# Joining the two parts of x on VectorE before the residual's transposing passes

## The chip, the cores and the metric

The kernel runs on one core of a Trainium2 chip. The metric is the device time of one execution in microseconds. Each number below is from the runs of this kernel or from one profiled execution of it.

## What is computed

Three blocks follow each other: a recurrence over 768 positions (8 heads of 48), a mixing block and a gated convolution block. Only the second one's first half matters here. x is the output of the recurrence, 768 positions by 384 features, for each of 4 batches:

```python
xt = x.transpose(0, 2, 1)
h = np.maximum(xt @ w_tok1, 0.0) @ w_tok2
u = x + h.transpose(0, 2, 1)
h2 = np.maximum(u @ w_ch1, 0.0) @ w_ch2
return u + h2
```

All of it is float32. The kernel gets float32 accuracy out of the faster fp32r products by splitting a tensor into a high part (the value rounded to fp32r) and a low part (what was rounded off): a product is high by high, high by low and low by high, three passes in the place of one.

## The kernel before, in words

TensorE (PE) does all products, ScalarE (ACT) writes high parts, VectorE (DVE) writes low parts, GpSimd (POOL) does the recurrence's states, SyncE (SP) issues loads. Each engine walks the same hand-written list of words, `PROGRAM`: a prologue, a `TRIP` that runs for b = 1, 2, 3, and a `TAIL`. A trip holds the recurrence of batch b beside the dense blocks of batch b - 1, so four batches of dense work lie in trips 1, 2, 3 and the tail. The order on each engine is fixed by that list; semaphores hold an engine at an instruction until another has done its part.

Words that matter here:

- `Z:s` writes x of one super unit (256 positions) to `xs`, high part by ACT and low part by DVE (L614). `xs` is [128, 2, 6, 384]: positions on the partitions, part, position block, feature.
- `G1.0.g` (g = 0, 1): the first product of batch b (`token_products`, L816). ACT and DVE then write the parts of `h1` (on DVE it is L619, tile h).
- `U.j.0` (j = 0, 1, 2, a tile of 256 positions): u transposed, features on the partitions, in three feature blocks `dt`. PE does for each `dt` 6 products of `h1` and the weight `tok2` (tiles tok,h) and then adds the residual: 4 transposing matmuls by the identity (tiles ident,xs), one for each of two position blocks and each of the two parts of x (L847 to L851). Feature blocks 0 and 1 share a PSUM bank, 2 has the next one; `mm_done` is raised after blocks 1 and 2. ACT then writes the high part of `us` (n = 0 for blocks 0 and 1, n = 1 for block 2) and DVE its low part (L632).
- `C1.j.g`, `C2.j.g` (g = 0..5): the two products with `ch1` and `ch2`, with the low part of `hid` by DVE (L619) between them. `C1.j.0` uses the PSUM bank that `U.j`'s n = 0 used, so PE can't begin it before DVE has written `us` low for n = 0 (`ring_free`).
- `X.j.0`: u + h2 into `xf` (DVE L647, L651, L653) and its parts `x2s` (ACT, DVE L657). `tap`, `gate`, `V`, `M`, `S`, `O`: the third block; DVE L670 does the taps, `V` is a product on PE, `M` multiplies it with the gate on DVE (L539, gate) and has ACT write a high part, `S` is DVE's low part, `O` the last product on PE (tiles outw,x2s), which needs both.
- `L1` to `L32`, `T`: levels of the recurrence. PE does 64 small products (tiles rk); DVE then scales r and k (L539, tiles rk or rk_next, called the scaling step below) and writes `at` (L594). PE's next level of the same super unit waits for the scaling step.

Around the change the list reads: in a trip `... G1.0.0 tap.2.1 tap.2.2 G1.0.1 V.2.0 tap.2.3 gate.2.0 M.2.0 tap.2.4 ... L4:3 O.2.0`, then at the start of the next one `L8:0 U.0.0 L16:0 C1.0.0 L32:0`; in its middle `X.0.0 L8:1 U.1.0 L16:1 C1.1.0 tap.0.0 L32:1`; later `X.1.0 U.2.0 T:2 tap.1.0 C1.2.0`. In the tail there are no levels: `U.0.0 C1.0.0`, `X.0.0 U.1.0 tap.0.0 tap.0.1 C1.1.0`, `X.1.0 U.2.0 tap.1.0 tap.1.1 C1.2.0`. The first `G1` (batch 0) stands at the end of the prologue.

Of the kernel before, what the change touches and what calls it, by code (L numbers as in the profile page):

```python
# [12 lines left out]
DM = H * D  # L13
# [174 lines left out]
def build(nc, rk, v, w, u, mask_d, ident_d, tok1_d, tok2_d, ch1_d, ch2_d, val_d, conv_d, outw_d, y_out):  # L188
    ctx = ExitStack()
    with ctx:  # L190
        def sb(name, shape, dt=F32):
            return ctx.enter_context(nc.sbuf_tensor(name, shape, dt))

        def sem(name):
            return ctx.enter_context(nc.semaphore(name))
# [35 lines left out]
        with ExitStack() as early:  # L231
            homes += [home_of_a_super_unit(early, 1), home_of_a_super_unit(early, 2)]
        xs = sb("xs", [P, 2, UNITS, DM], F32R)
        h1 = sb("h1", [P, 2, FT // P, DM], F32R)
# [38 lines left out]
        y_half, y_done = sem("y_half"), sem("y_done")  # L273
        xh_done, xl_done = sem("xh_done"), sem("xl_done")
        mm_done = sem("mm_done")
        ring_free = [sem("ring_free0"), sem("ring_free1")]
# [23 lines left out]
        def ring_filled(use):  # L300

            return use + 1
# [234 lines left out]
        def _(dve):  # L537
# [59 lines left out]
            def att(s, name):  # L597
# [12 lines left out]
                elif name == "Z":  # L610
# [5 lines left out]
                        .then_inc(xl_done, 1)  # L616

            def relu_low(out, bank, hi):
                return nc.vector.scalar_tensor_tensor(out, bank, 0.0, hi.bitcast(F32), ALU.max, ALU.subtract)  # L619

            def dense(b, kind, j, g):
                if kind == "G1":
                    use = RING_USE[(b, "G1", 0, g)]
                    need(dve, h1_hi, since(b, 2, g + 1))
                    relu_low(h1[:, LO, g, :], ps[:, RING + use % 2, 0:DM], h1[:, HI, g, :])\
                        .then_inc(ring_free[use % 2], 1)
                elif kind == "U":
                    for n, dts in ((0, slice(0, 2)), (1, slice(2, 3))):
                        use = RING_USE[(b, "U", j, n)]
                        need(dve, u_hi, since(b, 2 * TILES, 2 * j + n + 1))  # L630
                        bank = ps[:, RING + use % 2, 0:(2 - n) * TT].rearrange("p (d t) -> p d t", t=TT)
                        nc.vector.tensor_tensor(us[:, LO, dts, :], bank, us[:, HI, dts, :].bitcast(F32),  # L632
                                                ALU.subtract).then_inc(ring_free[use % 2], 1)
                elif kind == "C1":
                    use = RING_USE[(b, "C1", j, g)]
# [59 lines left out]
        def _(pe):  # L695
# [131 lines left out]
            def dense(b, kind, j, g):  # L827
# [7 lines left out]
                elif kind == "U":  # L835
                    ready = RING_USE[(b, "G1", 0, 1)]
                    need(pe, ring_free[ready % 2], ring_read(ready))
                    for dt in range(DT):
                        if dt == 2:
                            use = RING_USE[(b, "U", j, 1)]  # L840
                            need(pe, ring_free[use % 2], ring_read(use - 2))
                        bank = ps[:, RING + use % 2, dt % 2 * TT:(dt % 2 + 1) * TT]
                        rows = (lambda a, kt: h1[:, a, kt, dt * P:(dt + 1) * P],
                                lambda a, kt: wcols("tok2", a, kt * S + j * TT, TT))
                        hi_terms(bank, range(FT // P), *rows, True, True)
                        lo_terms(bank, range(FT // P), *rows, True, False)
                        for sc in range(2):  # L847
                            for part in (HI, LO):
                                ins = mm(bank[:, sc * P:(sc + 1) * P],
                                         xs[:, part, 2 * j + sc, dt * P:(dt + 1) * P].bitcast(F32), ident[:, :],  # L850
                                         False, is_transpose=True)  # L851
                        if dt:
                            ins.then_inc(mm_done, 1)
                elif kind == "C1":
# [136 lines left out]
```

## Time and profile before

| | |
|---|---|
| median of 3 runs | 670.53 us (670.13 to 674.12) |
| the profiled execution's own time | 670.57 us |
| its span, first to last instruction | 668.8 us |
| PE busy | 618.1 us (92%) |
| DVE busy | 390.7 us (58%) |
| ACT busy | 177.7 us (27%) |
| POOL busy | 97.0 us (15%) |
| mean granted TensorE clock | 0.990 |
| transposing matmuls on x | 144, from 99.3 to 618.2 us |

PEld is TensorE's weight load, which overlaps PE. Matmuls are pipelined, so the time that one takes from PE is the distance between the starts of neighbours and not its duration. A timeline row merges neighbours of one kind (x4 is four of them).

### The profile page before, as it was taken

What the parts mean: (1) busy time and instruction counts of PE and PEld (TensorE: products, weight loads), DVE (VectorE), ACT (ScalarE), POOL (GpSimd) and SP (SyncE); (2) the same over time, 40 slices, a digit from 0 to 9 for tenths busy, and PEclk for the clock granted to TensorE, in tenths of its full rate; (3) what the DMA queues carried; (4) which work ended last, traced back from release to release, by engine and by line L of the source; (5) the groups of instructions that cost most, each with busy time, mean ns of one, the idle gap of its engine ahead of it and who ended that gap; (6) DMA issues with size and microseconds to landing.
All of it is one profiled execution on the core that took longest, in us unless ns stands there. A gap on an engine that the chain in (4) does not pass through costs nothing.

```text
span 668.8 us, 24044 instructions
## 1 busy us (share of the span) xinstructions
PE 618.1 (92%) x11188; PEld 593.7 (89%) x11188; DVE 390.7 (58%) x609; ACT 177.7 (27%) x306; POOL 97.0 (15%) x110
## 2 busy tenths in 40 slices
PE   3588689999998999999998999999999999999995
PEld 2587679989998999999998999999999999999995
DVE  4894495495767284485768285385767152443524
ACT  2113324223232132122232132213222131222313
POOL 2214633303002000303003000403002000000000
PEclk9999989999999999999999999999999999999997
DMA  9811552400301200310400300210000000000000
GB/s 238 253 51 51 165 158 84 120 5 11 123 4 50 82 2 26 83 28 3 116 18 24 109 1 27 58 52 3 2 26 2 25 25 1 1 2 25 2 25 24
DMA packets 13331, 35.27 MB, mean 53 GB/s; under 512 B 1584, under 2 KB 7984, under 8 KB 11888
## 3 DMA queue, kind: packets, MB, share of 16 engines
q1 hardware_dynamic: 9776, 29.01, 15.6%
q10 hardware_dynamic: 3456, 4.72, 2.0%
q8 instruction: 88, 1.44, 0.9%
q14 instruction: 11, 0.09, 0.0%
HBM read 29.01 MB, written 4.72 MB: 50 GB/s over the span
## 4 chain that ended last, share of the span: by engine, by line
PE 79%; DVE 11%; issue 4%; ACT 2%; DMA 2%; POOL 1%; SPq 0%; DVEq 0%; ACTq 0%; POOLq 0%
PE ps L697 79%; DVE gate L670 3%; DVE at L594 2%; DMA w<-in_w_dram 2%; DVE rk L539 2%; DVE hid L619 1%; DVE wp L539 1%; DVE rk_next L539 1%; ACT x2s L429 1%; DVE us L632 1%; POOL st L412 1%; POOL st L415 1%; DVE xf L647 0%; DVE xf L651 0%; ACT hid L488 0%
## 5 line engine op out<-in xcount | busy, mean ns | idle before, releaser
L697 PE MATMUL ps<-us,ch 128*128 128x256 f32 x1296 | 167.1, 283 | 1.4 <-DVE us L632 0.8
L697 PE MATMUL ps<-hid,ch 128*128 128x256 f32 x1296 | 167.1, 283 | 0.0
L697 PEld LDWEIGHTS ps<-us,ch 128*128 128x128 f32 x1296 | 157.1, 188 | 4.8 <-DVE us L632 2.0
L697 PEld LDWEIGHTS ps<-hid,ch 128*128 128x128 f32 x1296 | 157.3, 188 | 1.9 <-issue 0.2
L619 DVE SCALAR_TENSOR_TENSOR hid<-ps,hid 128x512 fp32r<-128x512 f32 x72 | 49.8, 691 | 134.9 <-ACT hid L488 134.9
L488 ACT ACTIVATE hid<-ps 128x512 fp32r<-128x512 f32 x72 | 42.9, 597 | 153.5 <-PE ps L697 153.5
L594 DVE COPY_PREDICATED at<-masks,ps 128x512 f32<-128x512 uint8 (+1 forms) x72 | 65.3, 911 | 23.1 <-PE ps L697 23.1
L670 DVE SCALAR_TENSOR_TENSOR gate<-xf,cw,gate 128x256 f32<-128x256 f32 x144 | 73.1, 555 | 2.9 <-ACT gate L504 2.0
L697 PE MATMUL ps<-rk 48*64 48x32 f32 (+1 forms) x2240 | 48.8, 243 | 12.4 <-issue 8.8
L697 PEld LDWEIGHTS ps<-rk 48*64 48x64 f32 (+1 forms) x2240 | 44.9, 162 | 17.0 <-issue 14.7
L412 POOL TENSOR_TENSOR st<-st,wp 112x192 f32<-112x192 f32 x40 | 25.5, 638 | 207.5 <-ACT ds L429 200.8
L539 DVE TENSOR_TENSOR rk<-rk,wp 112x1024 f32<-112x1024 f32 x35 | 44.1, 1260 | 12.1 <-PE ps L697 12.1
L697 PE MATMUL ps<-x2s,val 128*128 128x256 f32 x324 | 41.6, 284 | 6.5 <-DVE hid L619 4.9
L697 PE MATMUL ps<-outw,x2s 128*128 128x384 f32 x216 | 43.1, 355 | 4.4 <-ACT x2s L429 4.4
L697 PEld LDWEIGHTS ps<-x2s,val 128*128 128x128 f32 x324 | 39.9, 191 | 7.4 <-DVE hid L619 5.6
L697 PEld LDWEIGHTS ps<-outw,x2s 128*128 128x128 f32 x216 | 39.6, 200 | 5.0 <-DVE gate L539 4.7
L539 DVE TENSOR_TENSOR rk_next<-rk_next,wp 112x1024 f32<-112x1024 f32 x25 | 30.9, 1235 | 12.1 <-PE ps L697 12.1
L697 PE MATMUL ps<-tok,h 128*128 128x256 f32 x216 | 34.3, 294 | 0.6 <-DVE h L619 0.5
L429 ACT ACTIVATE x2s<-xf 128x512 fp32r<-128x512 f32 (+1 forms) x24 | 11.3, 516 | 69.5 <-DVE xf L651 69.5
L697 PE MATMUL ps<-fk 48*64 48x64 f32 x768 | 18.2, 252 | 11.9 <-DMA ident<-in_ident_dram 9.9
L697 PEld LDWEIGHTS ps<-tok,h 128*128 128x128 f32 x216 | 28.0, 189 | 1.2 <-issue 0.6
L697 PEld LDWEIGHTS ps<-rk_next 48*64 48x64 f32 (+1 forms) x1600 | 23.8, 129 | 5.9 <-issue 3.8
(72 smaller groups left out, 614.1 us busy)
## 6 DMA issues: line engine op xcount, KB each, us to landing
rk<-in_rk_dram SPq DMA_DIRECT2D x7, 896.0 KB, 6.6
vs<-in_v_dram SPq DMA_DIRECT2D x12, 384.0 KB, 7.4
out_dram<-gate ACTq DMA_DIRECT2D x24, 192.0 KB, 3.6
rk_next<-in_rk_dram SPq DMA_DIRECT2D x5, 896.0 KB, 6.1
w<-in_w_dram SPq DMA_DIRECT2D x7, 448.0 KB, 7.9
gate<-in_moe_w_ch_dram SPq DMA_DIRECT2D x6, 384.0 KB, 3.3
xf<-in_moe_w_ch_dram SPq DMA_DIRECT2D x6, 384.0 KB, 3.2
w_next<-in_w_dram SPq DMA_DIRECT2D x5, 448.0 KB, 7.7
```

Source lines behind the costliest of these rows:

```text
L412: nc.gpsimd.tensor_tensor(new, now, decay[:, :, q].unsqueeze(2).to_broadcast([RD, PAIRS, D]), ALU.mult).then_inc(st_decayed, 1)
L415: nc.gpsimd.tensor_tensor(new, new, ds[0:RD, q], ALU.add).then_inc(st_done, 1)
L429: return nc.scalar.activation(out, in_, ACT.Copy)
L488: nc.scalar.activation(hid[:, HI, g % 2, :], ps[:, RING + use % 2, :], ACT.Relu)\
L539: return nc.vector.tensor_tensor(out, a, b_, ALU.mult)
L594: nc.vector.copy_predicated(out, may.unsqueeze(1).to_broadcast(list(out.shape)), src)\
L619: return nc.vector.scalar_tensor_tensor(out, bank, 0.0, hi.bitcast(F32), ALU.max, ALU.subtract)
L632: nc.vector.tensor_tensor(us[:, LO, dts, :], bank, us[:, HI, dts, :].bitcast(F32), ALU.subtract).then_inc(ring_free[use % 2], 1)
L670: nc.vector.scalar_tensor_tensor(gate3[:, dt, :], xf[:, dt, k:k + TT], cw[:, dt, k:k + 1], gate3[:, dt, :], ALU.mult, ALU.add).then_inc(ta ...
L697: return nc.tensor.matmul(out, lhsT, rhs, start=start, stop=stop, skip_group_check=True, **kw)
```

## The change

`x_sum` is a float32 tensor of [128, 6, 384] that gets the same place in SBUF as the high part of `xs`. A new function `join_x(b, j)` writes one third of it (2 position blocks, 128x768 elements) on DVE as high part plus low part; it waits for the last product of `G1`, which reads the high part. Piece 0 is done right behind `G1.0.1`'s low part, pieces 1 and 2 right behind the low parts of `U.0.0` and `U.1.0`: 12 additions in all. In `U` the products of both feature blocks of a bank come first and the transposing matmuls behind them, one per position block on `x_sum` in the place of two on `xs`: 72 in the place of 144. PE waits for the piece (`x_joined`) before the transposing matmuls.

```diff
+        with ExitStack() as joined:
+            x_sum = joined.enter_context(nc.sbuf_tensor("x_sum", [P, UNITS, DM], F32))
         xs = sb("xs", [P, 2, UNITS, DM], F32R)
...
+            def join_x(b, j):
+
+                dve.wait_ge(mm_done, ring_filled(RING_USE[(b, "G1", 0, 1)]))
+                units = slice(2 * j, 2 * j + 2)
+                nc.vector.tensor_tensor(x_sum[:, units, :], xs[:, HI, units, :].bitcast(F32),
+                                        xs[:, LO, units, :].bitcast(F32), ALU.add).then_inc(x_joined, 1)
...
                     relu_low(h1[:, LO, g, :], ps[:, RING + use % 2, 0:DM], h1[:, HI, g, :])\
                         .then_inc(ring_free[use % 2], 1)
+                    if g == 1:
+                        join_x(b, 0)
...
                         nc.vector.tensor_tensor(us[:, LO, dts, :], bank, us[:, HI, dts, :].bitcast(F32),
                                                 ALU.subtract).then_inc(ring_free[use % 2], 1)
+                    if j + 1 < TILES:
+                        join_x(b, j + 1)
...
-                    for dt in range(DT):
-                        if dt == 2:
-                            use = RING_USE[(b, "U", j, 1)]
+                    for n, dts in enumerate((range(2), range(2, DT))):
+                        use = RING_USE[(b, "U", j, n)]
+                        if n:
                             need(pe, ring_free[use % 2], ring_read(use - 2))
...
-                        hi_terms(bank, range(FT // P), *rows, True, True)
-                        lo_terms(bank, range(FT // P), *rows, True, False)
-                        for sc in range(2):
-                            for part in (HI, LO):
-                                ins = mm(bank[:, sc * P:(sc + 1) * P],
-                                         xs[:, part, 2 * j + sc, dt * P:(dt + 1) * P].bitcast(F32), ident[:, :],
-                                         False, is_transpose=True)
-                        if dt:
-                            ins.then_inc(mm_done, 1)
...
+                            hi_terms(banks[dt], range(FT // P), *rows, True, dt == dts[0])
+                            lo_terms(banks[dt], range(FT // P), *rows, True, False)
+                        need(pe, x_joined, since(b, TILES, j + 1))
+                        for dt in dts:
+                            for sc in range(2):
+                                ins = mm(banks[dt][:, sc * P:(sc + 1) * P], x_sum[:, 2 * j + sc, dt * P:(dt + 1) * P],
+                                         ident[:, :], False, is_transpose=True)
+                        ins.then_inc(mm_done, 1)
```

Three places show what moves. The first is PE at `U.0.0` of batch 0, between the products of `L8:0` and `L16:0` (tiles rk_next). Before:

```order
87 L697 MATMUL ps<-tok,h 128x256 [waits ring_free0,ring_free1,w_lo1,w_lo0]
88 L697 MATMUL ps<-tok,h 128x256 x5
89 L697 MATMUL ps<-ident,xs 128x128 x4
90 L697 MATMUL ps<-tok,h 128x256 x6
91 L697 MATMUL ps<-ident,xs 128x128 x4
92 L697 MATMUL ps<-tok,h 128x256 [waits ring_free1]
93 L697 MATMUL ps<-tok,h 128x256 x5
94 L697 MATMUL ps<-ident,xs 128x128 x4
95 L697 MATMUL ps<-rk_next 64x32 [waits next_done8,into_done_L2]
```

The same place on PE now:

```order
87 L712 MATMUL ps<-tok,h 128x256 [waits ring_free0,ring_free1,w_lo1,w_lo0]
88 L712 MATMUL ps<-tok,h 128x256 x11
89 L712 MATMUL ps<-ident,x_sum 128x128 [waits x_joined]
90 L712 MATMUL ps<-ident,x_sum 128x128 x3
91 L712 MATMUL ps<-tok,h 128x256 [waits ring_free1]
92 L712 MATMUL ps<-tok,h 128x256 x5
93 L712 MATMUL ps<-ident,x_sum 128x128 [waits x_joined]
94 L712 MATMUL ps<-ident,x_sum 128x128
95 L712 MATMUL ps<-rk_next 64x32 [waits next_done8,into_done_L2]
```

Of 12 transposing matmuls 6 are left, and the first group of them stands behind 12 products and a new wait.

The second place is DVE in a trip, at `G1.0.1` and the taps, `M` and `S` of the third block behind it. Before:

```order
326 L619 SCALAR_TENSOR_TENSOR h<-ps,h 128x384 [waits h1_hi]
327 L670 SCALAR_TENSOR_TENSOR gate<-xf,cw,gate 128x256
328 L670 SCALAR_TENSOR_TENSOR gate<-xf,cw,gate 128x256 [waits tap_done]
329 L539 TENSOR_TENSOR gate<-ps,gate 128x512 [waits mm_done,gate_done]
330 L670 SCALAR_TENSOR_TENSOR gate<-xf,cw,gate 128x256 [waits tap_done] x2
331 L681 TENSOR_TENSOR x2s<-gate,x2s 128x512 [waits gv_hi]
```

Now:

```order
332 L630 SCALAR_TENSOR_TENSOR h<-ps,h 128x384 [waits h1_hi]
333 L626 TENSOR_TENSOR x_sum<-xs 128x768 [waits mm_done]
334 L685 SCALAR_TENSOR_TENSOR gate<-xf,cw,gate 128x256
335 L685 SCALAR_TENSOR_TENSOR gate<-xf,cw,gate 128x256 [waits tap_done]
336 L543 TENSOR_TENSOR gate<-ps,gate 128x512 [waits mm_done,gate_done]
337 L685 SCALAR_TENSOR_TENSOR gate<-xf,cw,gate 128x256 [waits tap_done] x2
338 L696 TENSOR_TENSOR x2s<-gate,x2s 128x512 [waits gv_hi]
```

The addition of piece 0 stands ahead of the taps and of `M`'s multiplication (gate<-ps,gate).

The third place is DVE at `U.1.0` of a trip. Before:

```order
243 L632 TENSOR_TENSOR us<-ps,us 128x512 [waits u_hi]
244 L632 TENSOR_TENSOR us<-ps,us 128x256 [waits u_hi]
245 L539 TENSOR_TENSOR rk_next<-rk_next,wp 112x2x32x16 [waits decay_done16,lev_done16]
246 L539 TENSOR_TENSOR wp<-wp 112x16 [waits decay_done32,st_done]
247 L594 COPY_PREDICATED at<-masks,ps 128x32x16 [waits into_done_L8]
```

Now:

```order
248 L645 TENSOR_TENSOR us<-ps,us 128x512 [waits u_hi]
249 L645 TENSOR_TENSOR us<-ps,us 128x256 [waits u_hi]
250 L626 TENSOR_TENSOR x_sum<-xs 128x768 [waits mm_done]
251 L543 TENSOR_TENSOR rk_next<-rk_next,wp 112x2x32x16 [waits decay_done16,lev_done16]
252 L543 TENSOR_TENSOR wp<-wp 112x16 [waits decay_done32,st_done]
253 L598 COPY_PREDICATED at<-masks,ps 128x32x16 [waits into_done_L8]
```

The addition of piece 2 stands ahead of the scaling step of `L16:1`, for which PE's products of `L32:1` wait.

## Rows read from the trace of the kernel before

**Rows 1.** The page: its span, and busy time of each engine.

```profile
span 668.8 us, 24044 instructions
PE 618.1 (92%) x11188; PEld 593.7 (89%) x11188; DVE 390.7 (58%) x609; ACT 177.7 (27%) x306; POOL 97.0 (15%) x110
```

**Rows 2.** The chain that ended last, at U.1.0 of trip 3: start, us, what.

```profile
441.26 1.23 DVE rk L539
...
449.34 69.89 PE ps L697 x1339
```

**Rows 3.** Timeline at the first U.0.0: start, us, engine, line, operation, out<-in.

```profile
98.25 3.04 POOL L384 TENSOR_TENSOR ch<-xf,ch 128x768 fp32r<-128x768 f32 x1 [5.98 <-ACT ch L429]
98.28 1.21 DVE L539 TENSOR_TENSOR rk_next<-rk_next,wp 112x1024 f32<-112x1024 f32 x1
98.46 0.77 PEld L697 LDWEIGHTS ps<-tok,h 128*128 128x128 f32 x6 [0.60 <-issue]
...
99.18 0.46 PEld L697 LDWEIGHTS ps<-ident,xs 128*128 128x128 f32 x4
...
99.61 0.77 PEld L697 LDWEIGHTS ps<-tok,h 128*128 128x128 f32 x6
...
102.12 1.02 PEld L697 LDWEIGHTS ps<-rk_next 48*64 48x64 f32 x64 [0.17 <-issue]
```

**Rows 4.** Groups by shape: busy us, mean ns of one, idle before.

```profile
L697 PE MATMUL ps<-ident,xs 128*128 128x128 f32 x144 | 21.6, 272 | 0.0
...
L647 DVE TENSOR_TENSOR xf<-us 128x768 f32<-128x768 f32 x12 | 11.5, 958 | 1.0
```

**Rows 5.** Timeline around U.1.0 of trip 3.

```profile
448.60 1.01 DVE L632 TENSOR_TENSOR us<-ps,us 128x512 fp32r<-128x512 f32 x2
449.34 2.18 PEld L697 LDWEIGHTS ps<-us,ch 128*128 128x128 f32 x18 [0.18 <-DVE us L632]
...
449.54 1.21 DVE L539 TENSOR_TENSOR rk<-rk,wp 112x1024 f32<-112x1024 f32 x1
...
451.65 0.65 PEld L697 LDWEIGHTS ps<-rk 48*32 48x32 f32 x64
```

**Rows 6.** Timeline around U.2.0 of trip 3.

```profile
497.81 1.11 DVE L632 TENSOR_TENSOR us<-ps,us 128x512 fp32r<-128x512 f32 x2
497.96 1.02 PEld L697 LDWEIGHTS ps<-ident,rk_next 48*64 48x64 f32 x64 [0.17 <-issue]
...
499.04 2.18 PEld L697 LDWEIGHTS ps<-us,ch 128*128 128x128 f32 x18
```

**Rows 7.** Timeline at U.0.0 of the tail.

```profile
551.32 0.60 ACT L429 ACTIVATE us<-ps 128x512 fp32r<-128x512 f32 x1 [2.19 <-PE ps L697]
...
552.70 4.33 PEld L697 LDWEIGHTS ps<-us,ch 128*128 128x128 f32 x36 [0.49 <-DVE us L632]
```

**Rows 8.** Timeline behind G1.0.1: the end of trip 2, then of trip 3.

```profile
395.41 0.55 DVE L619 SCALAR_TENSOR_TENSOR h<-ps,h 128x384 fp32r<-128x384 f32 x1
...
395.87 1.00 DVE L670 SCALAR_TENSOR_TENSOR gate<-xf,cw,gate 128x256 f32<-128x256 f32 x2
396.79 0.68 DVE L539 TENSOR_TENSOR gate<-ps,gate 128x512 f32<-128x512 f32 x1
...
397.60 0.63 ACT L429 ACTIVATE x2s<-gate 128x512 fp32r<-128x512 f32 x1 [1.45 <-PE ps L697]
...
398.56 3.10 PEld L697 LDWEIGHTS ps<-outw,x2s 128*128 128x128 f32 x18
...
545.17 3.11 PEld L697 LDWEIGHTS ps<-outw,x2s 128*128 128x128 f32 x18 [0.99 <-DVE gate L539]
```

**Rows 9.** Timeline of DVE behind U.0.0 of trip 3.

```profile
407.91 1.23 DVE L539 TENSOR_TENSOR rk_next<-rk_next,wp 112x1024 f32<-112x1024 f32 x1 [0.33 <-PE ps L697]
```

**Rows 10.** Timeline of POOL, then of DVE, in the prologue.

```profile
83.59 2.54 POOL L384 TENSOR_TENSOR ch<-xf,ch 128x768 fp32r<-128x768 f32 x1
...
84.37 2.31 DVE L539 TENSOR_TENSOR wp<-w_next 112x512 f32<-112x512 f32 x1
```

More of the change, by code:

```diff
@@ L274, in build @@
         xh_done, xl_done = sem("xh_done"), sem("xl_done")
+        x_joined = sem("x_joined")
         mm_done = sem("mm_done")
@@ L837, in dense @@
                     need(pe, ring_free[ready % 2], ring_read(ready))
-                    for dt in range(DT):
-                        if dt == 2:
-                            use = RING_USE[(b, "U", j, 1)]
+                    for n, dts in enumerate((range(2), range(2, DT))):
+                        use = RING_USE[(b, "U", j, n)]
+                        if n:
                             need(pe, ring_free[use % 2], ring_read(use - 2))
-                        bank = ps[:, RING + use % 2, dt % 2 * TT:(dt % 2 + 1) * TT]
-                        rows = (lambda a, kt: h1[:, a, kt, dt * P:(dt + 1) * P],
-                                lambda a, kt: wcols("tok2", a, kt * S + j * TT, TT))
-                        hi_terms(bank, range(FT // P), *rows, True, True)
-                        lo_terms(bank, range(FT // P), *rows, True, False)
-                        for sc in range(2):
-                            for part in (HI, LO):
-                                ins = mm(bank[:, sc * P:(sc + 1) * P],
-                                         xs[:, part, 2 * j + sc, dt * P:(dt + 1) * P].bitcast(F32), ident[:, :],
-                                         False, is_transpose=True)
-                        if dt:
-                            ins.then_inc(mm_done, 1)
+                        banks = {dt: ps[:, RING + use % 2, dt % 2 * TT:(dt % 2 + 1) * TT] for dt in dts}
+                        for dt in dts:
+                            rows = (lambda a, kt: h1[:, a, kt, dt * P:(dt + 1) * P],
+                                    lambda a, kt: wcols("tok2", a, kt * S + j * TT, TT))
+                            hi_terms(banks[dt], range(FT // P), *rows, True, dt == dts[0])
+                            lo_terms(banks[dt], range(FT // P), *rows, True, False)
+                        need(pe, x_joined, since(b, TILES, j + 1))
+                        for dt in dts:
+                            for sc in range(2):
+                                ins = mm(banks[dt][:, sc * P:(sc + 1) * P], x_sum[:, 2 * j + sc, dt * P:(dt + 1) * P],
+                                         ident[:, :], False, is_transpose=True)
+                        ins.then_inc(mm_done, 1)
                 elif kind == "C1":
```

## The prediction

> **What bounds the kernel now.** I read the page first. PE is busy 618.1 of 668.8 us, DVE 390.7 [rows 1]: the change takes work from the engine that is nearly full and gives it to the one that isn't. Whether that pays is not in the shares, because PE walks a fixed list and stops wherever a DVE result is late. So the second view is the chain that ended last. Most of it is PE, but in the middle of each trip it leaves PE: from 441.26, the scaling step of L4:1, DVE carries it for 8 us through X.0.0 and the low parts of U.1.0, and only at 449.34 does PE take over [rows 2]. PE time saved inside such a stretch buys nothing. The third view is the timeline at each U and each G1, because every part of the change stands there.
>
> **What is taken from PE.** At the first U.0.0, 6 products start at 98.46, the 4 transposing matmuls at 99.18, the next products at 99.61 [rows 3]. So 4 passes take 0.43 us of PE, 0.107 each. The mean of 272 ns [rows 4] is the length of a pipelined pass, not its price. Two passes fewer in each of three feature blocks is 0.215 x 3 = 0.645 us per U, and 12 U give 7.7 us. That is the ceiling; what arrives depends on what PE meets next.
>
> - U.0.0 in trips 2 and 3: L16:0 and C1.0.0 follow and are not waited for, so 2 x 0.65 = 1.3 us arrive.
> - U.1.0 in the trips: C1.1.0 starts at 449.34 behind an idle time that DVE's us ends, and DVE got there from its own queue (the low parts run from 448.60 without idle time before them) [rows 5]. PE would only wait 0.65 longer. 3 x 0.
> - U.2.0 in the trips: T:2 starts at 497.96 and C1.2.0 at 499.04. DVE begins the two low parts at 497.81, straight from X.1.0, and the first ends about 0.7 later, near 498.50 [rows 6]. PE could be there at 498.39 but has to wait for that, so about 0.5 arrives, 3 x 0.5 = 1.5 us.
> - The tail's three U: nothing stands between U and C1, and C1.0.0 idles 0.49 for the first low part, which follows ACT's 0.60 from 551.32 [rows 7]. That line starts when feature block 1 is done, so only blocks 0 and 1 count: 0.43 each, 1.3 us. The saving in block 2 lengthens the wait.
> - U.0.0 of trip 1: 0.65, if the addition ahead of it does no harm (next part).
>
> **What is given to DVE.** The trace has the same operation: an addition of the two parts of us, 128x768, at 958 ns [rows 4]. Neighbours on DVE overlap by almost 0.1 (a start at 395.41 with 0.55, the next start at 395.87 [rows 8]), so an addition takes about 0.9 of DVE's time, 12 x 0.9 = 11 us in all. By place:
>
> - Behind U.0.0 in the trips (3 times). The scaling step of L16:0 starts at 407.91 after DVE was idle 0.33 for PE [rows 9]. C1.0.0 starts with it on PE, the products of L32 come 2.3 later (as from 449.34 to 451.65 [rows 5]), and the step takes 1.23, so it has 1.1 of room. It comes 0.9 - 0.33 = 0.55 later, so I take 0. In the tail DVE idles behind U.0.0: 0.
> - Behind U.1.0 in the trips (3 times). The scaling step of L16:1 is first in line at 449.54 and takes 1.21 [rows 5]. With 0.9 ahead of it, it ends at about 451.6, and PE wants it at 451.65. No room is left, none is lost. I take 0, with 0.9 each as the price if it is 0.9 later than this. In the tail DVE waits for ACT's taps there: 0.
> - Behind G1.0.1 at the ends of trips 1, 2 and 3. Here the addition stands ahead of two taps and of M's multiplication at 396.79 (0.68). ACT's copy waits for that multiplication, O.2.0 for the copy. Now M ends at 397.47, ACT starts at 397.60 and ends at 398.23, and O starts at 398.56 [rows 8]: 0.13 and 0.33 of room. Of 0.9 us later about 0.45 reaches O's start, and its low-part products wait for S, which comes 0.9 later too with less room. Bounds 0.45 and 0.9; I take 0.65 for trips 1 and 2. In trip 3 no level stands ahead of O, and it already idles 0.99 (it starts at 545.17) [rows 8], so only the first room is there: 0.8. Together 2.1 us.
> - Behind the first G1.0.1. The addition takes the place of the scaling step at 98.28, which started just as POOL's weight subtraction did (98.25). POOL's took 3.04 us, ending at 101.29: it stood until DVE's 1.21 were over and then ran about 1.8 [rows 3]. When DVE came second, it was DVE that stood: POOL's subtraction from 83.59 took 2.54, ending at 86.13, and a DVE step of half the size that began at 84.37 took 2.31 and ended 0.55 behind it [rows 10]. So POOL slips in between two DVE instructions. Then the addition runs to 99.24, POOL to 101.04, the scaling step to 102.25, where PE wants it for L16:0 at 102.12 - 0.65 = 101.47 [rows 3]. Behind it follow the step into at, 0.7, and the first low part of us, 0.7, so C1.0.0 starts near 103.6 in the place of 102.12 + 1.06 = 103.18. The 0.65 gained turns into about 0.4 lost. If POOL doesn't slip in, the gain stays. I take the loss.
>
> The Trainium skill, page "SBUF — State Buffer", section "Who interferes with whom", says of this pair that a VectorE instruction with two SBUF inputs contends with a GpSimd instruction that reads SBUF, and that the first one holds the pair for all of it. By that rule the trace's 3.04 and 2.31 are one mechanism, and the join, with both inputs in SBUF, is exposed to it while M's multiplication, with one input in PSUM, is not. The sum by the rule is the sum by the rows.
>
> No join is waited for by PE itself: at the first U it ends at 99.24, and the first transposing pass now stands 12 products behind 98.46, at 99.9 [rows 3]. Elsewhere it is done long before.
>
> **Sum.** -1.3 - 1.5 - 1.3 + 2.1 + 0.4 = -1.6 us against the profiled execution's 670.57, which is 0.04 from the median of 670.53. That gives 669.0 us.
>
> **The rivals.**
> (a) The likeliest, 669.0, own range 667.6 to 670.6: chance 0.70.
> (b) DVE has the room: POOL doesn't slip in and the additions behind G1 reach O with nothing. Then -0.65 in the place of +0.4, and no 2.1: 670.57 - 4.75 = 665.8. For it speaks that DVE is busy only 58%; against it that O already waits for DVE in one of the three places. With the stretches that DVE paces freed as well the ceiling is 670.57 - 7.7 = 662.9. Together 0.12, of which 0.03 for less than 663.9.
> (c) Slower: the additions ahead of the scaling steps of L16. The point that decides is 451.65: if the scaling step of L16:1 ends later, PE's L32:1 waits, then L32's own scaling step and the low part of hid behind it. At U.1.0 the room is about 0.05 by my numbers. If 0.9 shows at each of the three, 669.0 + 2.7 = 671.7; if at the three U.0.0 as well, 674.4. For it speaks that there is no room; against it that it would take an addition longer than those of us. Chance 0.16, of which 0.04 for more than 677.3, which needs the additions to meet POOL there too.
> (d) A pass is worth its 272 ns: 72 x 0.272 = 19.6 us, 651.0. Against it stands the 0.43 for four [rows 3], and that PE can't have 144 x 0.272 = 39 us in 21.6 us of busy time [rows 4]. Chance 0.02.
>
> For (d) there is a rule: the page "TensorE: Matmul & The Clock Gate" of the Trainium skill, section on PE-mode transpose, gives about 275 ns for a 128x128 transpose in a kernel (bf16). The trace's 272 ns agrees with it as a length, and its 0.107 us from start to start doesn't as a cost.
>
> **How the numbers follow.** About 1% (6.7 us) is what a measurement of this kernel can tell from no change. Within 1% is 663.9 to 677.3, which takes (a), (c) and most of (b): 0.91. Faster by over 1%: 0.05, the end of (b) and (d). Slower by over 1%: 0.04. The range leaves out about one in ten on each side: below the middle of (b)'s 665.8 and (a)'s 667.6, at 666.4, and above (c)'s first step, at 671.8.
>
> **What would show it.** U's own length on PE: 3.45 us now (three times 0.72 + 0.43), 2.8 after. C1.1.0 of the trips ended by DVE's us as now, with a longer idle time; the DVE stretch from L4:1 to there still on the chain. L32:1's products within 0.1 of their place behind C1.1.0. O.2.0 at the ends of the trips with idle time for ACT's x2s or DVE's gate where the first two now have none. At the first U.0.0, the first scaling step 1.8 longer, with POOL's subtraction across it. The additions at 0.96, one longer if (a) has the order of the port the other way round. The prediction is wrong if a transposing pass behind its like costs other than 0.107 us, if a satisfied wait on PE costs something, or if products of two feature blocks back to back are slower than 0.12 us each.

## The result and the profile after

The changed kernel takes 666.61 us (median of 19 runs, 664.66 to 670.3), the kernel before beside it 670.4 (19 runs). The ratio is 0.9943, with a 95% interval of 0.9927 to 0.9959: 3.8 us or 0.57% less, between 0.41% and 0.73%. The forecast was 669.0, with a range from 666.4. The sign was right, and the gain is more than twice what the sum said. The profiled execution took 665.62 us for itself.

The page, lines as in [rows 1], and the chain's shares by engine (before: PE 79%, DVE 11%):

```profile
span 663.5 us, 23912 instructions
PE 609.6 (92%) x11116; PEld 584.6 (88%) x11116; DVE 401.4 (60%) x621; ACT 177.1 (27%) x306; POOL 98.2 (15%) x110
...
PE 70%; DVE 18%; issue 4%; ACT 3%; DMA 2%; POOL 1%; DVEq 1%; SPq 0%; ACTq 0%; POOLq 0%
```

PE has 8.5 us less, DVE 10.7 more, and DVE's share of the chain has grown: part of what U saves is now a wait for DVE. The two new groups by shape (busy us, mean ns):

```profile
L712 PE MATMUL ps<-ident,x_sum 128*128 128x128 f32 x72 | 11.8, 272 | 0.0
L626 DVE TENSOR_TENSOR x_sum<-xs 128x768 f32<-128x768 f32 x12 | 11.4, 948 | 0.0
```

PE at U.0.0 of trip 3 (start, us, engine, line, operation, out<-in):

```profile
401.81 1.49 PEld L712 LDWEIGHTS ps<-tok,h 128*128 128x128 f32 x12
403.24 0.46 PEld L712 LDWEIGHTS ps<-ident,x_sum 128*128 128x128 f32 x4
403.67 0.79 PEld L712 LDWEIGHTS ps<-tok,h 128*128 128x128 f32 x6
...
404.81 1.02 PEld L712 LDWEIGHTS ps<-rk_next 48*64 48x64 f32 x64 [0.17 <-issue]
405.88 2.20 PEld L712 LDWEIGHTS ps<-us,ch 128*128 128x128 f32 x18
408.21 0.65 PEld L712 LDWEIGHTS ps<-rk_next 48*32 48x32 f32 x64
```

Four passes take 403.67 - 403.24 = 0.43 us, the two of the last block 0.24, and U itself 404.64 - 401.81 = 2.83 in the place of 3.45. The small products of L32 begin 2.33 behind C1.0.0, before it was 2.31: the addition behind U.0.0 costs next to nothing.

The place of [rows 5], U.1.0 of trip 3, PE and then DVE:

```profile
445.31 1.05 PEld L712 LDWEIGHTS ps<-rk 48*64 48x64 f32 x64 [0.84 <-issue]
446.54 2.20 PEld L712 LDWEIGHTS ps<-us,ch 128*128 128x128 f32 x18 [0.18 <-DVE us L645]
448.94 0.67 PEld L712 LDWEIGHTS ps<-rk 48*32 48x32 f32 x64 [0.20 <-issue]
...
445.81 1.01 DVE L645 TENSOR_TENSOR us<-ps,us 128x512 fp32r<-128x512 f32 x2
446.74 0.94 DVE L626 TENSOR_TENSOR x_sum<-xs 128x768 f32<-128x768 f32 x1
447.61 1.22 DVE L543 TENSOR_TENSOR rk<-rk,wp 112x1024 f32<-112x1024 f32 x1
```

What U saves turns into idle time ahead of L16:1 (0.84), C1.1.0 still starts behind DVE's us, and the scaling step ends at 448.83, where PE is ready at 448.74 (its 0.20 of idle time began there). L32:1 comes 2.40 behind C1.1.0, before it was 2.31.

The place of [rows 8], behind G1.0.1 at the end of trip 1 (PE, DVE, ACT), and O.2.0 at the end of trip 3:

```profile
246.98 3.14 PEld L712 LDWEIGHTS ps<-outw,x2s 128*128 128x128 f32 x18 [0.66 <-issue]
...
243.68 0.95 DVE L626 TENSOR_TENSOR x_sum<-xs 128x768 f32<-128x768 f32 x1
...
245.46 0.68 DVE L543 TENSOR_TENSOR gate<-ps,gate 128x512 f32<-128x512 f32 x1
...
246.24 0.63 ACT L433 ACTIVATE x2s<-gate 128x512 fp32r<-128x512 f32 x1 [2.28 <-DVE gate L543]
...
542.74 3.14 PEld L712 LDWEIGHTS ps<-outw,x2s 128*128 128x128 f32 x18 [1.81 <-DVE gate L543]
```

And the first U.0.0, the place of [rows 3], POOL and DVE:

```profile
99.17 3.92 POOL L388 TENSOR_TENSOR ch<-xf,ch 128x768 fp32r<-128x768 f32 x1 [5.98 <-ACT ch L433]
...
99.20 0.95 DVE L626 TENSOR_TENSOR x_sum<-xs 128x768 f32<-128x768 f32 x1
100.07 1.22 DVE L543 TENSOR_TENSOR rk_next<-rk_next,wp 112x1024 f32<-112x1024 f32 x1
```

POOL waited for both DVE instructions here, and the scaling step took its ordinary 1.22.

**Where 5.2 us of span went.** I compare the two traces at the same instruction of PE and take the difference of the starts. The prologue is 0.94 longer in this execution (first U.0.0 at 99.40, before 98.46). From there to C1.0.0 of the tail it was 454.24, now 450.45: -3.79. To the start of the last O another -1.23, and from the start of the last O to the end of the span it is 7.88 in the place of 9.03. Of the 3.79, 1.93 are three short stops of PE that only before has; the other 1.86 are left for the sum's terms. One is 0.18 at 327.33; the two large ones stand in the run of small products (A, L1, B of the recurrence) in the middle of trips 2 and 3. Before:

```profile
277.52 0.36 PEld L697 LDWEIGHTS ps<-st,rk 48*64 48x64 f32 x13 [0.79 <-issue]
...
429.51 0.43 PEld L697 LDWEIGHTS ps<-st,rk_next 48*64 48x64 f32 x16 [0.96 <-issue]
```

Nothing in these runs waits for another engine; the change doesn't touch them and stands 15 us away or more. Trip 1 has such a stop in both. Before, 8 products are left behind it (125.22, 0.95; the row of weight loads says x7, because the eighth product's load came ahead of the stop), after, one load and two products:

```profile
125.65 0.13 PEld L712 LDWEIGHTS ps<-st,rk_next 48*64 48x64 f32 x1 [0.95 <-issue]
```

### The profile page after: what moved, and what is told of

The parts are those of the page before. It is cut to its first block, busy times and chain, and to the rows that moved or that the text cites. A ratio compares the mean times of both kernels' runs of the same rounds, so it can differ in the third digit from the quotient of the medians.

```text
span 663.5 us, 23912 instructions
## 1 busy us (share of the span) xinstructions
PE 609.6 (92%) x11116; PEld 584.6 (88%) x11116; DVE 401.4 (60%) x621; ACT 177.1 (27%) x306; POOL 98.2 (15%) x110
## 3 DMA queue, kind: packets, MB, share of 16 engines
q10 hardware_dynamic: 3456, 4.72, 2.0%
HBM read 29.01 MB, written 4.72 MB: 51 GB/s over the span
## 4 chain that ended last, share of the span: by engine, by line
PE 70%; DVE 18%; issue 4%; ACT 3%; DMA 2%; POOL 1%; DVEq 1%; SPq 0%; ACTq 0%; POOLq 0%
PE ps L712 70%; DVE gate L685 5%; DVE at L598 2%; DVE rk L543 2%; DMA w<-in_w_dram 2%; ACT x2s L433 1%; DVE rk_next L543 1%; DVE x2s L672 1%; DVE wp L543 1%; DVE xf L666 1%; DVE xf L662 1%; DVE us L645 1%; DVE hid L630 1%; POOL st L416 1%; POOL st L419 1%
## 5 line engine op out<-in xcount | busy, mean ns | idle before, releaser
L712 PEld LDWEIGHTS ps<-outw,x2s 128*128 128x128 f32 x216 | 38.2, 194 | 7.5 <-DVE gate L543 5.6
L712 PE MATMUL ps<-tok,h 128*128 128x256 f32 x216 | 31.4, 290 | 0.6 <-DVE h L630 0.5
L712 PEld LDWEIGHTS ps<-fk 48*64 48x64 f32 x768 | 16.3, 163 | 14.5 <-DMA ident<-in_ident_dram 10.0
```

Of the source, the lines that this page charges most:

```text
L712: return nc.tensor.matmul(out, lhsT, rhs, start=start, stop=stop, skip_group_check=True, **kw)
```

## The experiments

Two questions: what each addition costs in its place, and whether the 1.75 us of vanished stops belong to the change. For the second my theory was that such a stop belongs to a place in PE's instruction stream: it comes at a fixed period of instructions, and shows only where they are used up fast (64 small products take 1.02 us, 18 large ones 2.2). The change leaves out 12 instructions in each U and so moves everything behind. The rival was chance, or the DMA traffic of the moment.

### No addition

```diff
-                    if g == 1:
-                        join_x(b, 0)
...
-                                ins = mm(banks[dt][...], x_sum[:, 2 * j + sc, ...], ident[:, :], False, is_transpose=True)
+                                ins = mm(banks[dt][...], xs[:, HI, 2 * j + sc, ...].bitcast(F32), ident[:, :], False, is_transpose=True)
```

> The changed kernel without the 12 additions on VectorE and without the wait for them; the residual takes its one transposing pass from the high part of x, so the low part is left out of it. TensorE's instructions are those of the changed kernel. Theory A (the additions cost about 2.1 us behind the three G1.0.1 and next to nothing elsewhere; the rest of the -3.8 us is TensorE's): about 664.4 us, 2.2 below the changed kernel's 666.6, ratio to before 0.991; in its trace O.2.0 at the ends of trips 1 and 2 starts without idle time. Rival B (the additions are hidden everywhere): 666.6, as the changed kernel. Rival C (they also cost behind U.0.0 and U.1.0): 662 or less.

Measured: ratio 0.9888 (0.9863 to 0.9914), 663.53 us. From the first U.0.0 to C1.0.0 of the tail 448.50, 1.95 less than after. O.2.0 has no idle time in trips 1 and 2 and 0.98 in trip 3. So by the two traces the 12 additions, 11.4 us of DVE, cost about 2 us of time. The medians say 3.1 (663.53 and 666.61), and the next two experiments show the same gap between trace and medians; what the traces don't place stays open.

### The addition behind G1 later

Piece 0's addition moves behind the scaling step of L4:3 in trips 1 and 2, and behind the last S in trip 3.

```diff
+                    if m == 4 and s % SUPERS == 0 and s >= 2 * SUPERS:
+                        join_x(s // SUPERS - 1, 0)
...
-                    if g == 1:
+                    if g == 1 and b == 0:
                         join_x(b, 0)
...
+                    if (b, j, g) == (B - 2, 2, 1):
+                        join_x(b + 1, 0)
```

> The changed kernel with only piece 0's addition moved for batches 1 to 3: behind the scaling step and mask of L4:3 in trips 1 and 2 (VectorE is idle about 1 us there) and behind the last S of the third block in trip 3. TensorE's instructions are unchanged. Theory A: the 2.1 us behind G1.0.1 come back, 664.5 us, ratio to before 0.991, the same time as the kernel without any addition; O.2.0 of trips 1 and 2 starts as L4:3's products end. Rival B: 666.6, no difference.

Measured: ratio 0.9891 (0.986 to 0.9923), 662.67 us. The end of trip 2, PE and then DVE:

```profile
397.11 1.02 PEld L716 LDWEIGHTS ps<-rk_next 48*64 48x64 f32 x64
398.18 3.10 PEld L716 LDWEIGHTS ps<-outw,x2s 128*128 128x128 f32 x18
...
401.69 0.95 DVE L628 TENSOR_TENSOR x_sum<-xs 128x768 f32<-128x768 f32 x1
```

O.2.0 follows L4:3 without idle time. The time is not above that of the kernel without additions, so nearly all that they cost is this one place, three times. In this execution POOL did slip in, as the prediction had it:

```profile
101.11 2.33 POOL L388 TENSOR_TENSOR ch<-xf,ch 128x768 fp32r<-128x768 f32 x1 [7.51 <-ACT ch L433]
...
101.68 2.85 DVE L543 TENSOR_TENSOR rk_next<-rk_next,wp 112x1024 f32<-112x1024 f32 x1
```

From U.0.0 to C1.0.0 it is then 5.05 us, where before it was 4.72 and after 4.07.

### All additions of the trips out of the way

As the last one, and pieces 1 and 2 behind the low part of C1.0.1.

```diff
-                    if j + 1 < TILES:
-                        join_x(b, j + 1)
...
+                    if (j, g) == (0, 1):
+                        join_x(b, 1)
+                        join_x(b, 2)
```

> All additions but the very first where VectorE is idle: piece 0 as in the second experiment, pieces 1 and 2 behind the low part of C1.0.1, where VectorE waits over 2 us. TensorE's instructions are those of the changed kernel. Theory A: the 0.2 us by which L32:1 comes later behind U.1.0 in each trip go as well, so about 0.3 to 0.6 us less than the second experiment's kernel, 662.2, if no POOL instruction gets between the first addition and L8:0's scaling step; if one does, 663.2.

Measured: ratio 0.9898 (0.9871 to 0.9926), 663.3 us; not to be told from the last one, and not the 662.2 that was expected, although POOL didn't get in between here (C1.0.0 4.07 behind U.0.0). U.0.0 to C1.0.0 of the tail 448.51, as without any addition. L32:1 of trip 3 has lost its idle time:

```profile
444.52 2.21 PEld L717 LDWEIGHTS ps<-us,ch 128*128 128x128 f32 x18 [0.19 <-DVE us L647]
446.86 0.65 PEld L717 LDWEIGHTS ps<-rk 48*32 48x32 f32 x64
```

2.34 behind C1.1.0: the addition behind U.1.0 had made L32:1 0.06 to 0.09 later. It doesn't go further: from C1.1.0 to U.2.0 the three trips take 44.95, 44.97 and 44.99 us here and 44.97, 44.99 and 44.98 in the last experiment.

### Only the order of products

The kernel before, with the products of both feature blocks of a bank first and then 8 and 4 passes on `xs`: no addition, no pass less.

```diff
-                    for dt in range(DT):
+                    for n, dts in enumerate((range(2), range(2, DT))):
...
+                        for dt in dts:
+                            for sc in range(2):
+                                for part in (HI, LO):
```

> The kernel before with the products of both feature blocks of a bank first and the transposing matmuls behind them; all 144 of them, on both parts of x, and no addition. TensorE has as many instructions as before and at the same places but inside U. Theory A (the order inside U is worth nothing): 670.4, ratio 1.000 within 0.002, U's length on TensorE 3.45 us as before, and the three gaps in the runs of small products as before. Rival F (fewer changes between the two kinds of matmul are worth some of the gain): 2 to 3 us less.

Measured: ratio 0.9994 (0.9969 to 1.002). PE in U.0.0 of the tail:

```profile
547.66 1.49 PEld L697 LDWEIGHTS ps<-tok,h 128*128 128x128 f32 x12 [0.44 <-ACT gate L429]
549.10 0.90 PEld L697 LDWEIGHTS ps<-ident,xs 128*128 128x128 f32 x8
```

8 passes in 0.86 (the next products start at 549.96): again 0.107 each. The stops are where they were before, at the 8th, 13th and 16th product from the end (1.31, 0.58 and 0.96); the instruction count is the same too. In the tail, U.0.0 to U.1.0 takes 29.32 against 29.60 before. The 0.3 lies between C1.0.0 and U.1.0: 25.62 to 25.63 in the three profiles with the old order, 25.33 or 25.34 in all ten with the new one. It comes with the order alone; why stays open.

### Moving the stream without the change

52 calls of small products more in the prologue of the kernel before. Each call is two loads and two products in the trace, so that is 104 products and 208 instructions:

```diff
+            PADS = {(0, "L2"): 13, (0, "L4"): 13, (0, "L8"): 13, (0, "L16"): 13}
+                for _ in range(PADS.get((s, name), 0)):
+                    mm(ps[0:CH, RING, 0:CH // 2], ident[0:D, 0:CH], ident[0:D, 0:CH // 2], True)
```

> The kernel before with 52 small products by the identity added to TensorE's prologue, at four places where it waits for VectorE; they hold about 208 instructions and shift where every later instruction stands in TensorE's stream, and do nothing else. Theory D (the idle time of 0.8 to 0.96 us in the middle of the recurrence's small products of each trip, with no wait on a semaphore there, comes when a boundary of every 256 instructions of TensorE's stream falls late in that run; the changed kernel lost two of the three because it has fewer instructions): by my count the boundary is moved out of the run in all three trips, so the three gaps vanish and the span is 2 to 2.5 us shorter after the prologue, about 668.3 us. Rival E (the gaps come from the data or the semaphores there): the three gaps stay, 670.4.

Measured: all three stops are gone. U.0.0 to C1.0.0 of the tail is 451.40, before 454.24: -2.84, where the three stops were 0.95 + 0.79 + 0.96 = 2.70. A stop of 0.42 has come just behind trip 3's run (434.83). The median is worse all the same (674.5, ratio 1.0053, 1.0032 to 1.0075), because the prologue became 6.7 longer. So the kernel before can lose its stops without any part of the change.

21 such calls in the same places of the changed kernel, 84 instructions:

```diff
+            PADS = {(0, "L2"): 5, (0, "L4"): 5, (0, "L8"): 5, (0, "L16"): 6}
```

> The changed kernel with 21 such small products added to the prologue, about 84 instructions. Theory D: by my count the boundary comes back into the late part of the run of small products in trips 2 and 3 (about 62 and 32 instructions before its end), so gaps of 0.5 to 1 us appear there where the changed kernel has none, and the time is 1 to 2 us longer, about 668 us. Rival E: no gaps in trips 2 and 3, 666.6.

Measured: 674.67 us, ratio 1.0051 (1.0025 to 1.0076). The stop of trip 1 has gone from its place, and others have come:

```profile
180.74 0.36 PEld L712 LDWEIGHTS ps<-rk_next 48*64 48x64 f32 x17 [1.68 <-issue]
...
332.51 0.19 PEld L712 LDWEIGHTS ps<-rk 48*64 48x64 f32 x3 [1.12 <-issue]
...
435.89 0.43 PEld L712 LDWEIGHTS ps<-st,rk_next 48*64 48x64 f32 x16 [1.38 <-issue]
```

The last is where the count put it. The one expected in trip 2's run is there too, 31 products before the end, but has only 0.06 us (282.73). The first two stand in runs of other levels, which the expectation had not gone through. U.0.0 to C1.0.0 of the tail 454.85, 4.4 more than after. The POOL order of the second experiment (0.97) is in that.

12 such calls, 48 instructions, inside U.1.0 of trip 1 of the changed kernel:

```diff
+                        for _ in range(12 if (b, j, n) == (0, 1, 1) else 0):
+                            mm(ps[0:CH, RING + use % 2, 0:CH // 2], ident[0:D, 0:CH], ident[0:D, 0:CH // 2], True)
```

> The changed kernel with 12 small products by the identity (48 instructions) added to TensorE's stream inside U.1.0 of trip 1, where TensorE has 1.5 us to spare before L8:1's scaling step; they are overwritten by the next product. Nothing ahead of them moves. Theory D (a boundary every 256 instructions stalls TensorE when it falls near the end of the run A:0 L1:1 B:0): by my count the boundary now falls about 26 instructions, 13 small products, before the end of that run in trip 2 and just behind the run in trip 3, so a gap of about 0.8 us comes back in trip 2, at the last 13 products, and none in trip 3; from the first U to the end about 0.8 us longer than the changed kernel's 564.1. Rival E (the gaps depend on time or data and not on the place in the stream): no gap in trip 2.

Measured: 668.65 us, ratio 0.9983 (0.9955 to 1.0012). The stop of trip 2 is back, at the same 13th product from the end:

```profile
277.03 0.36 PEld L712 LDWEIGHTS ps<-st,rk 48*64 48x64 f32 x13 [0.99 <-issue]
...
428.79 1.94 PEld L712 LDWEIGHTS ps<-hid,ch 128*128 128x128 f32 x16 [0.82 <-issue]
```

In trip 3, where none was expected, one stands just behind the run. Trip 1's, ahead of the added products, is unmoved (0.95). U.0.0 to C1.0.0 of the tail: 453.03, 2.58 more than after, of which the stops are 0.99, 0.82 and a 0.52 at 174.22.

### Both kernels once more

> The changed kernel again, unaltered, for one more profiled execution. If the stalls belong to places in TensorE's stream, the runs of small products in trips 2 and 3 are again without a stall and trip 1 has its 0.95 at the last product (125.6). If POOL's place against the first addition is chance, the scaling step behind it may take 1.2 or 2.85 us; where POOL starts within 0.1 us of the addition or before it, 1.2. The last O takes 7.8 us where the granted clock stays up, 8.8 to 9.1 where it falls.

> The kernel before again, unaltered, for one more profiled execution. If the stalls belong to places in TensorE's stream, they are at the same products: 8, 13 and 16 from the end of the runs in trips 1, 2 and 3, with 0.6 to 1.3 us each. If they are chance, they are elsewhere. First U.0.0 to C1.0.0 of the tail 454.2 within 0.4.

Measured, first the changed kernel, then trips 2 and 3 of the one before, whose trip 1 has 0.83 at 124.28:

```profile
126.74 0.13 PEld L712 LDWEIGHTS ps<-st,rk_next 48*64 48x64 f32 x1 [1.50 <-issue]
```

```profile
276.34 0.36 PEld L697 LDWEIGHTS ps<-st,rk 48*64 48x64 f32 x13 [0.58 <-issue]
...
428.14 0.43 PEld L697 LDWEIGHTS ps<-st,rk_next 48*64 48x64 f32 x16 [0.96 <-issue]
```

The places repeat to the product, the sizes don't (0.58 and 0.79, 0.95 and 1.50). The other kernels whose PE stream is that of after up to there have the stop of trip 1 at the same place and none over 0.12 in trips 2 and 3 as well. U.0.0 to C1.0.0 of the tail is 453.67 for the kernel before and 451.13 for the changed one here, 2.5 apart in the place of 3.8. The last O took 4.6 us in both (7.9 to the end); the 9.03 of the first profile of before was no property of that kernel. The POOL subtraction waited for both DVE instructions again (99.79, 3.87; the addition at 99.77).

### A second addition behind U, and behind G1

```diff
                 if j:
+                    done.then_inc(first_join, 1)
+                    dve.wait_ge(first_join, 2 * b + j)
+                    done = nc.vector.tensor_tensor(x_sum[:, units, :], x_sum[:, units, :], x_sum[:, units, :], ALU.max)
```

> The changed kernel, with a second DVE instruction of the same shape (128x768, two SBUF inputs, the maximum of x_sum with itself, in place) behind each addition that stands behind a U: 8 in all, 6 of them in trips. TensorE's stream is the same instruction for instruction. It measures the rooms that the prediction read ahead of the scaling steps of L16. Theory (the rooms are as read): each second instruction costs DVE about 0.95 us. Behind U.0.0 in the trips 0.55 of 1.1 us of room was left by the addition, so 0.4 shows, three times; behind U.1.0 none was left, so 0.95 shows, three times; in the tail nothing. Together +4.0 us: first U.0.0 to C1.0.0 of the tail 454.5 in the place of 450.45, median about 670.6. Rival (DVE has more room than read, PE is late at the same places for other reasons): L16:1 and L32:1 keep their places behind C1.1.0, +1 us at most.

Measured: 672.13 us, ratio 1.0023 (0.9999 to 1.0048), 5.4 us more than after by the ratios, where 4.0 was expected. From the first U.0.0 to C1.0.0 of the tail it is 456.85, 6.40 more. The two L32 of trip 3:

```profile
413.57 2.20 PEld L718 LDWEIGHTS ps<-us,ch 128*128 128x128 f32 x18
416.57 0.67 PEld L718 LDWEIGHTS ps<-rk_next 48*32 48x32 f32 x64 [0.80 <-issue]
...
454.90 2.20 PEld L718 LDWEIGHTS ps<-us,ch 128*128 128x128 f32 x18 [0.18 <-DVE us L651]
458.29 0.67 PEld L718 LDWEIGHTS ps<-rk 48*32 48x32 f32 x64 [1.19 <-issue]
```

Behind U.1.0 the distance is 3.39 (2.40 after): 0.99 more, all of the second instruction and its wait. Behind U.0.0 it is 3.00 (2.33 after): 0.67 more, so only about 0.3 of room was left and not 0.55. Trip 1 has 3.21 there, and the first U.0.0 POOL in between (4.81 to C1.0.0, 0.74 more).

The same behind piece 0's addition at the ends of the trips (`if not j and b:`):

> The changed kernel, with the same second instruction behind piece 0's addition at the ends of trips 1, 2 and 3 alone. TensorE's stream is the same. Theory (no room is left behind the addition there: O.2.0 already idles for it): 0.95 each reaches O.2.0's start in full, +2.9 us, median about 669.4, O.2.0's idle time 1.6 in trips 1 and 2 and 2.75 in trip 3. Rival (part of a later O is given back by what stands behind it, since DVE's own queue and not O paces the next levels): O.2.0 idles as long, but the stretch to the next C1 grows by half of it or less, +1.5 us.

Measured: 671.06 us, ratio 1.0008 (0.9977 to 1.0038). O.2.0 idles 1.65, 1.65 and 2.80: 0.99 more each time, as expected. But from C1.0.0 of trip 1 to C1.0.0 of the tail it is 452.53 in the place of 446.38, 6.15 more and not 3. The other 3 are in O itself, in trips 2 and 3:

```profile
249.62 3.15 PEld L718 LDWEIGHTS ps<-outw,x2s 128*128 128x128 f32 x18 [1.65 <-DVE gate L544]
...
401.15 4.67 PEld L718 LDWEIGHTS ps<-outw,x2s 128*128 128x128 f32 x18 [1.65 <-DVE gate L544]
...
549.05 4.63 PEld L718 LDWEIGHTS ps<-outw,x2s 128*128 128x128 f32 x18 [2.80 <-DVE gate L544]
```

The windows over these O (us, PE busy, granted clock, DMA share, GB/s) show it:

```profile
249.00:253.00 4.00, 3.35 (x18) 1.00 0.00 0
...
401.00:405.00 4.00, 3.82 (x15) 0.65 0.00 0
```

The granted clock fell. And the first U.0.0 in this execution had POOL in front:

```profile
99.82 1.83 POOL L389 TENSOR_TENSOR ch<-xf,ch 128x768 fp32r<-128x768 f32 x1 [4.75 <-ACT ch L434]
...
99.93 2.53 DVE L627 TENSOR_TENSOR x_sum<-xs 128x768 f32<-128x768 f32 x1
...
102.51 0.42 PEld L718 LDWEIGHTS ps<-ident,x_sum 128*128 128x128 f32 x4 [0.90 <-DVE x_sum L627]
```

### Every stop in all thirteen profiles

The traces also tell where in PE's stream each stop stands, and when the blocks of the queue that the page calls "q8 instruction" arrived. I counted all records of PE ahead of the stop: weight loads, products and semaphore instructions. "84 more" is the changed kernel with 21 calls more, "48 more" the one with 12.

| stop | records ahead | remainder by 256 | block landed | PE went on |
|---|---|---|---|---|
| before, trip 1 | 5570 | 194 | 123.66 | 125.22 |
| before, trip 2 | 11201 | 193 | 276.24 | 277.52 |
| before, trip 3 | 16833 | 193 | 428.14 | 429.51 |
| 84 more | 13249 | 193 | 331.14 | 332.51 |
| 48 more | 7618 | 194 | 172.78 | 174.22 |
| 48 more | 16833 | 193 | 427.52 | 428.79 |

Behind 95 us there are 28 stops of 0.1 us or more without a releaser between two products of one kind, in the 13 profiles. All 28 have the remainder 193 or 194, whatever word stands there. The ones that the expectations did not have ("84 more" in other levels, "48 more" at 174.22 and 428.79) are among them. The queue's packets have 16 KB each and are as many as PE's records divided by 256, within one (before 22565 / 256 = 88.1 with 88 packets, after 87.6 with 87, with 208 more 88.96 with 89). PE passes such a place 930 times behind 95 us in the 13 profiles, and never sooner than 1.21 us after the queue's packet one before had landed (at the k-th such place the packet k - 1, which is the one in the table); at the 28 stops it went on 1.21 to 1.62 us after. So a stop is PE waiting for its next 256 instructions. In the long runs of small products the last such place had been passed only 2.7 to 3.6 us earlier; 256 instructions of them, 128 products, take 2 x 1.02 = 2.04 us without a stop.

## Why the prediction was right in its sign and short in its size

- **A pass costs 0.107 us.** Right: 0.43 for four passes in after, 0.86 for eight in the order experiment; U is 2.83 long, 2.8 was said.
- **U.0.0 of trips 2 and 3, -1.3.** Right. L16 behind the first of them moves from 254.71 to 254.45 although O.2.0, which it follows, came 0.37 later (246.64 and 247.01): 0.63 gained.
- **U.1.0, 0.** Right: C1.1.0 starts behind DVE's us in all trips, with 0.65 more idle time ahead of L16:1.
- **U.2.0, -0.5 each.** Right: from U.2.0's start to C1.2.0 it is -0.53, -0.54 and -0.53.
- **The tail, -0.43 each.** Right: from each U's start to its C1 it is -0.44, -0.43 and -0.42. Another -0.28 between C1.0.0 and U.1.0 comes with the order of products, which the sum didn't price.
- **Additions behind G1, +2.1.** Right: +0.63, +0.65 and +0.81 at O.2.0. With them moved, the stretch from C1.0.0 of trip 1 to that of the tail falls from 446.38 to 443.66, of which 0.3 is a shorter stop in trip 1.
- **Additions behind U, 0.** Right within 0.3: L32 comes 0.02 and 0.09 later, 0.3 in all, and moving these additions away ("All additions of the trips out of the way") gained nothing more. The room behind U.1.0 was read right (none). That behind U.0.0 was misread: the scaling step was taken to start with C1.0.0 (407.69), but starts at 407.91 and ends at 409.14, and L32 starts at 410.00, so the room was 0.86 and not 1.1, and about 0.3 and not 0.55 behind the addition. Rival (c) needed a longer addition, and it took 0.95.
- **The first U.0.0, +0.4: the mis-sized term.** In after's two profiles it is -0.65 and -0.66. The step that failed is "POOL slips in between two DVE instructions". It does when it comes 0.3 behind the first (three profiles; C1.0.0 is then 0.09 to 0.33 later than before, so the 0.4 was a fair price), it waits for both when it comes within 0.03 of it (four profiles), and it goes first when it comes 0.11 ahead (one profile; C1.0.0 is 0.28 later). The sum took the one order as certain from rows in which only one was to be seen. Also, "No join is waited for by PE itself" fails in the last of these orders (0.90).
- **What the sum didn't have at all**: the stops in the small products. -0.79, -0.96 and -0.18 in the first pair of profiles, as much as all of its own terms. The prediction looked at the places that the change touches, and left out that 12 instructions fewer in each U move all later ones against the blocks of 256 in which PE gets them. With -0.65 in the place of +0.4 the sum is -2.65, with the 1.93 of the stops -4.6; the medians say -3.8. Up to C1.0.0 of the tail, where the sum lacks the tail's last two terms, that is -1.8 - 1.9 = -3.7, and the two pairs of profiles have -3.8 and -2.5 there: the stops' sizes differ from one execution to the next. That 666.61 still lies inside the range, by 0.2 us, is luck in part: both things left out of the sum fell on the side of a gain.
- **Rival (b)**'s 665.8 is nearer to the median than 669.0, but not by its mechanism: the additions behind G1 did reach O.
- **The last O.** Its 1.15 us less in the profile are the granted clock of single executions and not the change: 0.50 over it before and 0.65 after, and in the second pair of profiles both took 4.6 us.

The stops' link to the position in the stream is shown: same place in each of three profiles with the old stream, gone with 208 instructions more, back at the same product with 48. The period of 256 and the wait for the block of instructions are shown too, by the remainders and the landing times in the section on all thirteen profiles. My own counts of the program had put the three stops of before at 209, 224 and 233 of 256, places that drift and that missed stops; counted by the trace's records they don't drift. After, the place in question falls 11 products behind the end of trip 2's run (278.27, 0.09 us of idle time) and 26 behind the end of trip 3's, among large products. What stays open is why a block's packet starts 0.5 us behind the last such place in one case and 3 in another (84 more, trip 1), and with it the size of a stop.

## What to carry to other kernels

Price an operation added to a less busy engine by its place in that engine's queue: of twelve equal additions the eight behind U cost at most 0.3 us together, the three ahead of M's multiplication 2.1, and one nothing or 1.0, and moving those three behind it gave 662.7 us (ratio 0.9891) against 666.6. Where a change alters the number of instructions on an engine that runs dense streams of small ones, look for stops without a releaser in the trace of before, count the engine's records ahead of them by 256, and see where the change puts these places. Allow some tenths of a per cent for the stops' coming and going either way. Do not carry one observed order of two engines at a shared port into a sum as certain; give it as two prices.

## What the hardware showed beyond that

**PE waits for its instructions.** Stops of up to 1.68 us without a releaser, mostly in runs where 64 small products take 1.02 us. All stand at one place in each 256 instructions, and end 1.21 to 1.62 us after a 16 KB packet of the instruction queue has landed.

**POOL and DVE with SBUF operands.** POOL's subtraction takes about 1.8 us alone (1.83 when it starts 0.11 ahead of DVE). Started within 0.03 of it (before 98.25, after 99.17) it waited for DVE, and where two such DVE instructions follow each other for both (3.92, 3.87). Started 0.30 behind it got in between (2.33), and the second DVE instruction took 2.85. The Trainium skill, page "SBUF — State Buffer", section "Who interferes with whom", says that the first of the two holds the pair for all of its instruction; the 2.53 of an addition with POOL 0.11 ahead, and the 2.85, agree. So do the scaling steps of 2.73 and 2.71 us in two kernels without additions, where POOL started 0.18 and 0.20 ahead. Why POOL passes over the gap between the two DVE instructions in the one case and takes it in the other stays open.

**The granted clock behind short idle times.** O.2.0 behind 0.66 and 1.81 us of idle time ran at 1.00 in after (3.14 us). With one more us of DVE ahead (idle time 1.65 and 2.80) it ran at 0.64 over the whole of O in trips 2 and 3 (4.67 and 4.63), and in trip 1 with the same 1.65 at 1.00. So a delay of 1 us cost 2.5 in two of three places. The last O of the kernel, behind 3.75 us of idle time, took from 3.11 (at 1.00) to 5.6 in different executions; in the profile of before its middle was granted half of full speed, the lower of the two levels (1.2 GHz):

```profile
660.00:664.00 4.00, 4.00 (x13) 0.50 0.00 0
```
